# Splitting the last thirteen bias stores of an attention and two-layer MoE kernel, with thirteen buffers

## What is computed

```python
scores = scale * np.matmul(q, k.transpose(0, 1, 3, 2))
psi_rel = np.log1p(np.abs(rel))                      # rel = i - j
psi_i = np.log1p(np.maximum(pos[:, None], 1.0))
x = (psi_rel / psi_i)[..., None]
h = np.maximum(x @ w1 + b1, 0.0)                     # 32 hidden units
scores = scores + (h @ w2).transpose(2, 0, 1)[None]  # w2: 32 x 8 heads
attn = softmax(scores); attn_out = attn @ v
h = max(x @ w1, x @ w2, x @ w3); x = h @ w_out       # 2304 tokens, 512 -> 768 -> 512
h = x @ w_in; g = where(h >= 1, h, where(h <= -1, 0, (h + 1)**2 / 4)); out = g @ w_out
```

## Time and profile before

| | us |
|---|---|
| median of 3 runs | 1012.89 |
| lowest, highest | 1012.41, 1014.35 |
| the profiled execution | 1012.26 |
| its span, first to last instruction | 1010.2 |

### The profile page before, as it was taken

One profiled execution on the slowest core, in us unless ns is written; L12 is line 12 of the kernel. 1 busy time (PEld: TensorE's weight loads), 2 busy tenths in 40 slices (PEclk: granted clock), 3 DMA queues, 4 the chain that ended last, 5 costly groups with the idle time before them and its releaser, 6 DMA issues.

```text
span 1010.2 us, 23289 instructions
## 1 busy us (share of the span) xinstructions
PE 987.5 (98%) x8832; PEld 895.8 (89%) x8832; DVE 611.6 (61%) x1509; ACT 508.4 (50%) x1032; POOL 366.3 (36%) x634
## 2 busy tenths in 40 slices
PE   6979999999999999999999999999999999999998
PEld 4557777777777999999999999999999999999998
DVE  8957667667683232314231315777777877778776
ACT  8968788787793321212121213555545444545543
POOL 1049888888874796887720000000000000000000
PEclk9989999999999999999999999999999999999999
DMA  5882534425311456446550056976666666666772
GB/s 126 256 257 59 154 73 106 125 49 157 98 34 58 139 168 235 170 178 215 210 228 0 0 220 234 354 251 191 223 198 208 218 200 214 195 216 188 224 219 73
DMA packets 122725, 169.71 MB, mean 168 GB/s; under 512 B 67072, under 2 KB 84736, under 8 KB 120960
## 3 DMA queue, kind: packets, MB, share of 16 engines
q1 hardware_dynamic: 122528, 168.37, 53.2%
q10 hardware_dynamic: 96, 0.00, 0.0%
HBM read 129.64 MB, written 38.70 MB: 167 GB/s over the span
## 4 chain that ended last, share of the span: by engine, by line
PE 79%; DVE 1%; DMA 0%; ACT 0%; issue 0%; DVEq 0%
PE ps L1285 22%; PE ps L1350 20%; PE ps L1376 17%; PE ps L1312 7%; PE ps L1236 5%; PE ps L1176 4%; PE ps L1197 2%; PE ps L1211 1%; PE ps L1150 1%; DMA w_all<-win_scratch 0%; DVE s_sb L936 0%; DVE tb L1112 0%; DVE g_lo L1127 0%; ACT tb L874 0%; ACT g_hi L888 0%
## 5 line engine op out<-in xcount | busy, mean ns | idle before, releaser
L1285 PE MATMUL ps<-x_hi,w_all 128*128 128x384 f32 x864 | 225.9, 335 | 1.2 <-ACT ta L820 1.2
L1350 PE MATMUL ps<-x_hi,w_all 128*128 128x256 f32 x1152 | 219.2, 283 | 0.8 <-DMA w_all<-win_scratch 0.8
L1350 PEld LDWEIGHTS ps<-x_hi,w_all 128*128 128x128 f32 x1152 | 184.8, 192 | 1.0 <-DMA w_all<-win_scratch 1.0
L1376 PE MATMUL ps<-w_all,g_hi 128*128 128x256 f32 x1008 | 184.6, 283 | 0.2 <-DVE g_lo L1127 0.2
L1350 PE MATMUL ps<-x_lo,w_all 128*128 128x256 f32 x576 | 163.0, 283 | 0.0
L1285 PEld LDWEIGHTS ps<-x_hi,w_all 128*128 128x128 f32 x864 | 156.7, 188 | 2.9 <-DVE xT L957 1.7
L1376 PEld LDWEIGHTS ps<-w_all,g_hi 128*128 128x128 f32 x1008 | 157.2, 192 | 0.4 <-DVE g_lo L1127 0.4
L936 DVE CUSTOM_DVE_ANT_0 s_sb<-ps,bias_h 128x576 f32<-128x576 f32 (+1 forms) x160 | 114.8, 753 | 69.9 <-PE ps L1176 52.1
L1285 PE MATMUL ps<-x_lo,w_all 128*128 128x384 f32 x432 | 144.3, 334 | 0.0
L1376 PE MATMUL ps<-w_all,g_lo 128*128 128x256 f32 x504 | 142.6, 283 | 0.0
L592 POOL TENSOR_SCALAR probs<-probs,row_inv 128x576 f32<-128x576 f32 (+1 forms) x160 | 120.2, 761 | 19.3 <-DVE row_inv L966 18.7
(11 more groups left out here) (119 smaller groups left out, 1821.4 us busy)
## 6 DMA issues: line engine op xcount, KB each, us to landing
w_all<-win_scratch SPq DMA_DIRECT2D x144, 512.0 KB, 4.4
wt_scratch<-w_all SPq DMA_DIRECT2D x8, 1792.0 KB, 6.8
bias_scratch<-p_t SPq DMA_DIRECT2D x36, 296.0 KB, 4.5
w_all<-wt_scratch SPq DMA_DIRECT2D x5, 1792.0 KB, 7.5
win_scratch<-w_all SPq DMA_DIRECT2D x8, 1024.0 KB, 6.5
raw<-in_moe_w_out SPq DMA_DIRECT2D x22, 256.0 KB, 7.1
w_all<-wt_scratch SPq DMA_DIRECT2D x12, 448.0 KB, 6.8
bias_h<-bias_scratch SPq DMA_DIRECT2D x16, 288.0 KB, 4.5
```

What stands on the lines that cost most here:

```text
L1285: last = pe.matmul(ps[:, bank, 0:BLK], w[:, at:at + P], x[:, kt, :], start=(kt == 0 and n == 0), stop=(kt == KT - 1 and n == 2))
L1350: last = pe.matmul(ps[:, n_bank(n), f * SBT:(f + 1) * SBT], w_all[:, at + lo:at + lo + P], x[:, s, :], start=(kt == 0 and i == 0), stop=(k ...
L1376: last = pe.matmul(ps[:, bank, 0:HD], x[:, n % 2, g * P:(g + 1) * P], w_all[:, at + lo:at + lo + HD], start=(j == 0 and m == 0), stop=(j = ...
```

## The change

- The columns of w2b are put in another order: w2 goes into a new tile w2c, and VectorE copies it into w2b, four small copies, before it makes nb1. Head 2a + b comes to place 4b + a, in PSUM and in bias_scratch, so that the two heads of the first pair are at places 0 and 4. TensorE waits for the copies (w2_ok).
- NB is 13 instead of 8. Six buffers lie in a new tile bias_x, seven in the second half of p_t; the fourth hidden buffer moves to the start of p_t. A copy waits for its buffer from supertile 13 on.
- Supertiles 0 to 22 are stored as before. Of supertiles 23 to 35 only the places 0 and 4 are stored at first (`store_two`, 32 rows of 592 values). Tile 2's loads come behind supertiles 29 and 30.
- When all ten loads of the first pair's bias have landed, SP stores supertiles 23 to 35 whole, and goes on with load_qk(3).
- The first copies to p_t wait for the last bias product alone; those of group 1 (tile 5, slot 8) wait for all stores, and SP waits for them before it loads the next pair's bias.
- The eight semaphore increments at the start of SP's program are dropped.

```diff
-        NB = 8
+        NBX, NBP = 6, 7
+        NB = NBX + NBP
+        FULL = NSUP - NB
...
+            w2c = sb("w2c", [P, H], c=att)
...
-            bias_o = p_t_flat[:, 0:NB * BW].rearrange("p (e y) -> p e y", e=NB)
+            p_flat = [p_t[:, e, :, :, :].rearrange("p h c j -> p (h c j)") for e in range(2)]
+            hid.append(p_flat[0][:, 0:G4 * LTW].rearrange("p (g c) -> p g c", g=G4))
...
+            bias_x = sb("bias_x", [P, NBX, BW], c=att)
+            bias_o = [bias_x[:, e, :] for e in range(NBX)] + [p_flat[1][:, e * BW:(e + 1) * BW] for e in range(NBP)]
...
         def _(sp):
-            for e in range(NB):
-                sp.sem_inc(bias_free[e], 16)
...
-            sp.wait_ge(w2b_zero, 1)
             for r in range(G4):
-                sp.dma_start(w2b[r * HID:(r + 1) * HID, r * H:(r + 1) * H], w2).then_inc(w2_in, 16)
+                sp.dma_start(w2c[r * HID:(r + 1) * HID, :], w2).then_inc(w2_in, 16)
...
-                x = bias_d[t * P:t * P + n, 2 * hp + h, :]
+                x = bias_d[t * P:t * P + n, H // 2 * h + hp, :]
...
+            def store_two(s):
+
+                sp.dma_start(skewed(s).rearrange("i (h r) -> i h r", h=H)[:, 0:H:H // 2, 0:BW],
+                             bias_o[s % NB][0:P:H // 2, :]).then_inc(bias_two[s % NB], 16)
+
+            def first_bias(h, t):
+
+                for s in range(t * P // SUP, min((t + 1) * P // SUP, NSUP)):
+                    if s < FULL:
+                        sp.wait_ge(bias_free[s % NB], 16 * (s // NB + 1))
+                    else:
+                        sp.wait_ge(bias_two[s % NB], 16)
                 load_bias(0, h, t)
 
             for s in range(NSUP):
-                store_bias(s)
+                copied(s)
+                if s < FULL:
+                    store_bias(s)
+                else:
+                    store_two(s)
...
-                if s % 8 in (6, 7) and 14 <= s < NSUP - 4:
-                    first_bias(s % 8 - 6, s // 8 - 1, s // 8 * 8)
+                if s in (14, 15, 22, 23):
+                    first_bias(s % 8 - 6, s // 8 - 1)
...
+                if s in (29, 30):
+                    first_bias(s - 29, 2)
             for t in range(T - 1, NT):
                 for h in range(2):
-                    first_bias(h, t, min((t + 1) * P // SUP, NSUP))
+                    first_bias(h, t)
+            for t in range(NT):
+                for h in range(2):
+                    sp.wait_ge(bias_in[h][t], 16 * (1 + h))
+            for s in range(FULL, NSUP):
+                store_bias(s)
...
+                if i == B - 1:
+                    for e in range(NB):
+                        sp.wait_ge(bias_free[e], stored(NSUP, e))
...
-                act.wait_ge(bias_free[e], 16 * (s // NB + 1))
+                if s >= NB:
+                    act.wait_ge(bias_free[e], 16 * (s // NB))
...
                 act.wait_ge(px_ps, u + 1)
                 if u == 0:
+                    act.wait_ge(bias_ps, NSUP)
+                if u == NT:
                     for e in range(NB):
                         act.wait_ge(bias_free[e], stored(NSUP, e))
...
+            dve.wait_ge(w2b_zero, 1)
+            dve.wait_ge(w2_in, 16 * G4)
+            for r in range(G4):
+                lanes = slice(r * HID, (r + 1) * HID)
+                dve.tensor_copy(w2b[lanes, r * H:(r + 1) * H].rearrange("k (b a) -> k b a", b=2),
+                                w2c[lanes, :].rearrange("k (a b) -> k b a", b=2)).then_inc(w2_ok, 1)
             dve.wait_ge(small_in, 16 * 2 * G4)
...
-            pe.wait_ge(w2_in, 16 * G4)
+            pe.wait_ge(w2_ok, G4)
```

More of the change, by code:

```diff
@@ L105, in build @@
             p_t = sb("p_t", [P, 2, 2, T, S], c=att)
-            p_t_flat = p_t[:, :, :, :, :].rearrange("p i e c j -> p (i e c j)")
-            bias_o = p_t_flat[:, 0:NB * BW].rearrange("p (e y) -> p e y", e=NB)
-            hid.append(p_t_flat[:, NB * BW:NB * BW + G4 * LTW].rearrange("p (g c) -> p g c", g=G4))
+            p_flat = [p_t[:, e, :, :, :].rearrange("p h c j -> p (h c j)") for e in range(2)]
+            hid.append(p_flat[0][:, 0:G4 * LTW].rearrange("p (g c) -> p g c", g=G4))
             tqk = sb("tqk", [P, 2, 3, NT * P], c=att)
@@ L155, in build @@
         w2b_zero = sem("w2b_zero")
-        small_in, w2_in = sem("small_in"), sem("w2_in")
+        small_in, w2_in, w2_ok = sem("small_in"), sem("w2_in"), sem("w2_ok")
         a_dve = sem("a_dve")
@@ L166, in build @@
         bias_free = [sem(f"bias_free{e}") for e in range(NB)]
+        bias_two = [sem(f"bias_two{e}") for e in range(NB)]
         bias_in = [[sem(f"bias_in{e}_{t}") for t in range(NT)] for e in range(2)]
@@ L244, in stored @@
         def stored(n, e):
-            return 16 * ((n - 1 - e) // NB + 2)
+            return 16 * ((n - 1 - e) // NB + 1)
         def hid_count(s):
@@ L389, in _, with copied @@
             load_qk(0)
-            def store_bias(s):
+            def copied(s):
                 if s == LAST:
@@ L395, in store_bias, with skewed @@
                     sp.wait_ge(bias_sb, min(s + 1, NSUP - 1))
+            def skewed(s):
                 skew = bias_f[s * SUP * H * RS:(s + 1) * SUP * H * RS + SUP].rearrange("(i x) -> i x", i=SUP)
[L397 to L403, removed]
+                return skew[:, 0:H * RS]
+            def store_bias(s):
+                sp.dma_start(skewed(s).rearrange("i (h r) -> i h r", h=H)[:, :, 0:BW],
+                             bias_o[s % NB]).then_inc(bias_free[s % NB], 16)
+            def store_two(s):
[7 more added lines that the diff above has]
+                        sp.wait_ge(bias_two[s % NB], 16)
                 load_bias(0, h, t)
             for s in range(NSUP):
-                store_bias(s)
+                copied(s)
[3 more added lines that the diff above has]
+                    store_two(s)
                 if s in (2, 3):
@@ L698, in bias_copy @@
                 act.wait_ge(bias_ps, s + 1)
-                act.wait_ge(bias_free[e], 16 * (s // NB + 1))
-                act.activation(bias_o[:, e, :].rearrange("p (c y) -> p c y", c=2), ps[:, at:at + 2, 0:HB],
+                if s >= NB:
+                    act.wait_ge(bias_free[e], 16 * (s // NB))
+                act.activation(bias_o[e].rearrange("p (c y) -> p c y", c=2), ps[:, at:at + 2, 0:HB],
                                ACT.Identity, scale=1.0 / SCALE, bias=nconst[:, col:col + 1]).then_inc(bias_sb, 1)
@@ L923, in bias_copy @@
                 dve.wait_ge(bias_ps, s + 1)
-                dve.wait_ge(bias_free[e], 16 * (s // NB + 1))
-                dve.tensor_scalar(bias_o[:, e, :].rearrange("p (c y) -> p c y", c=2), ps[:, at:at + 2, 0:HB],
+                if s >= NB:
+                    dve.wait_ge(bias_free[e], 16 * (s // NB))
+                dve.tensor_scalar(bias_o[e].rearrange("p (c y) -> p c y", c=2), ps[:, at:at + 2, 0:HB],
                                   1.0 / SCALE, nconst[:, 1:2], ALU.mult, ALU.add).then_inc(bias_dve, 1)
@@ L945, in copy_lower @@
                 if u == 0:
+                    dve.wait_ge(bias_ps, NSUP)
+                if u == NT:
                     for e in range(NB):
```

## The result

The changed kernel takes 1018.26 us (median of 6 runs, 1016.50 to 1018.75) against 1013.05 us of the kernel before in the same runs; the ratio is 1.0057, 95% interval [1.0046, 1.0068]. It is slower, by 4.7 to 6.9 us. Forecast were 1015.2 us and +2.3 us: the sign is right, the size is not.

A forecast was written before the change was run, and what follows sets the result against it. The prediction took TensorE as the bound. 0.7 us of lateness plus 1.6 for the clock gave +2.3 on the profiled 1012.26 us, 1014.6; the median, 0.63 above, was forecast at 1015.2 us, range 1010.3 to 1018.3.

The forecast's parts named there:

- What bounds the kernel: Whole kernel: TensorE, busy 98% of the span; only delays before 84 us, or a new stall behind it, count.
- The start: Hidden tiles wait for w2 and its copies: start at 7.5 against 5.69 us, bias stage shifted 1.75 us, nothing absorbing it.
- Thirteen buffers: End of bias stage: no copy waits for a store; VectorE's first addition at 59.15 instead of 60.09, 0.95 us gained.
- A quarter of 13 stores: SP's queue: tile 4's load issued at 64.8 instead of 69.80; TensorE gains 2.5 us, reaching slot 8 at 82.4.
- The thirteen full stores: SP, ahead of load_qk(3): 9.1 us of stores, q and k land at 85.6, TensorE stands 3.2 us, 0.7 later than before.
- The counter-check by bandwidth: Thirteen full stores: 13 x 303 kB at 351 GB/s take 11.2 us, less SP's 2.3 us lead, 8.9.
- the slow rival: Slot 8: stores at 294 GB/s or q and k held up; landing 88 to 89, stall 6 us, +5.1, 1018.0; chance 0.15.
- The clock: TensorE behind the slot 8 stall: the granted clock drops, costing 1.6 us of lost full-speed work.
- The sum: Whole kernel: 0.7 of lateness and 1.6 of clock make +2.3 us, 1014.6 profiled, 1015.2 as median.

## Why the prediction was right in direction and wrong in size

- **What bounds the kernel**: right. All of the 6.5 us of span lie ahead of the scores of slot 10.
- **The start**: hidden tiles at 7.83 for 7.5, TensorE's first supertile at 9.49 for 9.0. The claim that nothing behind it absorbs the shift was wrong: the last product began 1.05 us later (56.12 for 55.07), not 1.75. Before, VectorE waited 1.44 us for ScalarE in the middle of the stage, and I had not counted that as slack; in the changed kernel it waits 0.47 there. In the changed kernel the start costs nothing that can be measured (1018.07 against 1018.26 with part of it taken out), as the stall covers it.
- **Thirteen buffers**: right; first addition at 58.49 for 59.15, earlier by what the start cost less. That they gain no time without the split wasn't in the prediction; the run of the buffers alone showed it.
- **A quarter of 13 stores**: right in kind; tile 4's load at 64.99 for 64.8, TensorE at slot 8 at 81.95 for 82.4. That 64.99 is so near is luck: SP ended the store of supertile 22 at 47.74, 0.9 us ahead of the 48.6 forecast, and the stretch from there took 17.25 us for 16.2.
- **The thirteen full stores, the step that failed**. The place, the queue and the waiting instruction were right; the landing was 88.89 for 85.6. Term by term: the last bias load had landed and the first store was issued at 68.84 for 68.4 (+0.4); from the first store to the first q it took 11.46 us for 9.1, 0.88 a store for 0.70 (+2.4); first to last issue of q and k took 6.25 for 5.7 (+0.6), as the first two, right behind the stores, took 1.23 us each; landing 2.3 after the last issue for 2.4 (-0.1). That is 3.3 us, all of the miss in the landing. The term that was mis-sized is the 9.1 us. The 0.70 was the quickest of the rows of several stores; the same view had a row of five at 0.93 us each, shown below, which gives 12.1 for thirteen. The counter-check by bandwidth, which gave 8.9, had the lead right and the rate wrong. ScalarE's copy of tile 5 waits for the last store and starts at 85.22, 5.0 us behind the end of the issues at 80.26, so SP was over 2 us ahead of the landings, as assumed; the forecast had this at 81.6. With the 2.3 us of lead, 11.4 us of issue are 13.7 us of data for 13 x 303 kB, some 287 GB/s by this estimate, and not the 351 of the best 2 us. It is near the 294 of the slow rival, at 0.15, whose landing of 88 to 89 came true and whose price was nearly right; it should have been the forecast.
- **The clock**: mechanism right, size 2.7 for 1.6. TensorE went from the turn of slot 8 to the scores of slot 10 in 7.93 us (88.89 to 96.82) instead of 5.27 (84.90 to 90.17), with the clock low until about 94.5; I had taken the price from a stretch behind a stall of 2.2 us, and this one was 6.94. That stretch wasn't the only one either: in the kernel before the clock was also 0.61 from 68 to 72 us. With TensorE kept at work the span fell by 2.4 us. The Trainium skill (TensorE: Matmul & The Clock Gate, What's actually happening) says that activity releases the throttle. These two traces agree with it: the kernels differ in the 55 transposes in TensorE's idle time alone, and with them the clock is 1.00 from 88 to 92 us instead of 0.50. Other traces aren't explained by it, as said at the end.
- **The sum**: 88.89 - 84.90 = 4.0 and 2.7 are 6.7 us by the trace, against 0.7 and 1.6; the spans differ by 6.5, the medians by 5.2.

The row of five stores, from the same view of the kernel before as the earlier trace rows:

```profile
54.57 4.64 SPq L397 DMA_DIRECT2D bias_scratch<-p_t  x5
```

The list of DMA issues of the changed kernel gives the small stores a median of 2.4 and 2.8 us from issue to landing for 74 KB, against the 2.2 us estimated from the Trainium skill (DMA: Bandwidth & Descriptors, Anatomy of one DMA), whose figures are for DMAs that GpSimd issues, while these come from SP; the measurement decides. Its rule against splitting did not decide the case: thirteen small DMAs cost SP some 7 us of issue, and tile 4's load still came 4.8 us forward.

## What to carry to other kernels

When a change takes work off a queue "for later", find what stands behind the new place, and work out the slack of the first thing that is needed there; here it was 4.7 us, and the list 11.5. Don't price a burst by the quickest short row of issues: 0.70 us a store gave 9.1 us, the row of five 12.1, and 11.46 were measured. Even bytes over the best bandwidth of the trace (3.94 MB over 351 GB/s, 11.2 us) are a lower bound for the data, and here the last landing came later still. Once the list was cut to what frees a buffer, the loads that are needed next came ahead of the rest, and idle time of the queue was filled, the same idea, with the small copies on GpSimd, made the kernel 2.3 to 5.2 us faster instead of 5 us slower.

## What was not expected of the hardware

- Granted clock: in the kernel before with the later start, TensorE was at work 3.6 to 4.0 of every 4 us from 64 to 80 us and the clock stayed at 0.50 to 0.54 all the same; in the kernel before with thirteen buffers it was 0.50 to 0.52 from 60 to 76 us. In the changed kernel 3.09 of 4 us of work from 60 to 64 us were followed by 1.00; with the transposes, the same program up to there, 3.17 of 4 us were followed by 0.58. So the program doesn't decide it, nor does TensorE's work in the 4 us before tell these apart. What makes the difference was not found. In the two first traces some 2 us were lost beside it, as much as the shifts that were to be measured.
- Four copies of 32 x 8 values took 0.74 us on VectorE (`tensor_copy`) and 1.67 us on GpSimd (`tensor_scalar`).
